# Attention, routed experts and an ELU layer on one core: the finish step of a head moves from slot 4 to slot 5

## The chip, the cores and the metric

The kernel runs on one core of a Trainium2 chip. The metric is the device time of one execution in microseconds (us). The core has a matrix engine (TensorE, PE in the profile, its weight loads shown apart as PEld), a vector engine (VectorE, DVE), a scalar engine (ScalarE, ACT), GpSimd (POOL), and queues that start DMA transfers (SyncE, SP, and others). Each engine works through its own instruction list in order; they meet only at semaphores.

## The reference

Three layers follow one another. The changed lines lie in the first.

```python
q_bits = (np.einsum('bhsd,dk->bhsk', q, proj) > 0)       # 6 hash bits, likewise for k
mask = q_bucket[:, :, :, None] == k_bucket[:, :, None, :]
scores = np.where(mask, scale * np.matmul(q, k.transpose(0, 1, 3, 2)), -1e9)
attn = np.exp(scores - np.max(scores, axis=-1, keepdims=True))
attn = attn / (np.sum(attn, axis=-1, keepdims=True) + 1e-09)
x = np.matmul(attn, v)        # 2 x 8 heads, 768 rows, head width 64; then x is (1536, 512)
# routed layer: argmax over x @ w_gate picks one of 8 experts; relu(x @ w1[e]) @ w2[e], scaled
# last layer: h = x @ w_in; elu(h) @ w_out, 512 -> 2048 -> 512
```

## The kernel before

Attention runs over 16 heads, each of 6 tiles of 128 query rows against all 768 keys: 96 tiles, one per **slot**. Every engine walks the same list of slots: `body(i)` covers a pair of heads, twelve slots `s`, with `j = s // 6` the head of the pair, `u = s % 6` the slot within the head, and `h = i*2 + j`. Pair 0 and pair 7 are written out, pairs 1 to 6 run as a hardware loop, in which some addresses come from registers, and a last short call, `body(PAIRS)`, drains the pipeline. Values are kept as pairs of numbers, a high and a low part, so most products take two or three matmuls.

The work on one tile is spread over the slots. For the tile of slot `s` TensorE writes four score matmuls into `ps_s` (two buffers, lines 564, 565). VectorE finds the row maximum (956), GpSimd makes scale and bias of it in two small steps (432, 434), ScalarE writes `probs` with an exponential and collects the row sums (799). Two slots later TensorE transposes `probs` in two halves of three into `ps_t` (579); ScalarE copies each half to `pt_hi` (790), VectorE forms the low part `pt_lo` (969). `ps_t` has one buffer for each half, so the transposes of a slot wait for `lo_moved` of the slot before (576). The product with V (595, 596) follows for groups of three tiles, in the slots `u` = 5 and 0 and `u` = 2 and 3. ScalarE moves it to `o_sb` at the end of its slots `u` = 0 and `u` = 3 (807).

Beside that, each head prepares the next one through a single bank, `ps_p`: in `u` = 0 and `u` = 1 the next q and k are transposed (`turn_qk`, 529), moved by ScalarE (774) and VectorE (926); in `u` = 2 and 3 they are multiplied by the hash projection (`project`, 535 to 537) and turned to bits (930). The same bank serves the **finish step** of the head before: `finish_head(h - 1)` (twelve matmuls on line 544, two passes of each of six) multiplies `o_sb` by an identity with the gate weights beside it, and VectorE's `move_rows` (940, 942) scales the result by the inverse row sums `inv` into `logit_parts` and `x_rows`. The order of use of the bank is kept by `prep_moved`: each user waits until VectorE has moved what the user before it wrote. So `turn_qk` of `u` = 0 waits for `move_rows` (583). The inverse itself is taken by `reciprocal` (963), after GpSimd has added a small constant to the sums in `u` = 2 (444).

The order inside one slot matters. TensorE: scores, then `turn_qk` of u = 1 or `project`, then the six transposes, then `turn_qk` of u = 0, then the product with V, last the finish step. VectorE: maximum, moves of `ps_p`, `reciprocal`, the two low parts, last `move_rows`. ScalarE: move of q/k for u = 1, the two high parts, move for u = 0, the exponential, the copy to `o_sb`. `FINISH_AT` (244) names the slot of the finish step; `slots_of` (268) uses it for the length of the last short call. The finish step is done in the heads `h` = 1 to 15 for the head before, and once more at the end; heads 1 to 14 also prepare a next head.

After attention VectorE computes the routing, GpSimd scatters the rows, and the expert layer and the last layer follow, each dependent on the one before.

Of the kernel before, what the change touches and what calls it, by code (L numbers as in the profile page):

```python
# [20 lines left out]
def attention_moe_mlp(nc, q, k, v, proj, w_gate, w1, w2, w_in, w_out, out):  # L21
# [59 lines left out]
    with ExitStack() as ctx:  # L81
# [159 lines left out]

        RT_SHIFTED, RT_CHOSEN = 3, 7
        TURN_AT = [2, 5, 8, 11]
        FINISH_AT = 4
        CHUNKS = 4 + 4 * (HEADS - 1) + HEADS

        def chunks_before(h):

            if not isinstance(h, int):
                return h * 5 + 3  # L250
            return 4 if h == 0 else h * 5 + 3 - (4 if h == HEADS else 0)

        def live(i, s, lag, count, per=1):

            if not isinstance(i, int):
                return True
            n = i * SPP + s - lag
            return n >= 0 and n // per < count
# [8 lines left out]
        def slots_of(i):  # L267
            return range(FINISH_AT + 1 if isinstance(i, int) and i == PAIRS else SPP)

        def has_next(i, j):  # L270

            return not isinstance(i, int) or i * 2 + j + 1 < HEADS

        def has_last(i, j):

            return not isinstance(i, int) or i * 2 + j >= 1
# [246 lines left out]
        def _(pe):  # L523
# [24 lines left out]
            def body(i):  # L548
                for s in slots_of(i):
# [35 lines left out]
                    if live(i, s, 5, 2 * HEADS, 3) and (s - 5) % 3 < 2:  # L585
# [11 lines left out]
                        if part == 1:  # L597
                            last.then_inc(weighted, 1)
                    if u == FINISH_AT and has_last(i, j):
                        pe.wait_ge(prep_moved, chunks_before(h) + (4 if has_next(i, j) else 0))  # L600
# [319 lines left out]
        def _(dve):  # L920
            v_ = nc.vector

            def move_qk(j, h, half, bank):
                dve.wait_ge(qk_hi_moved, h * 2 + half + 1)
                cols = slice(half * HW, half * HW + HW)
                v_.tensor_tensor(qk_lo[j][:, cols], bank[:, 0:HW], qk_hi[j][:, cols].bitcast(F32), ALU.subtract).then_inc(prep_moved, 1)

            def move_bits(j, h, half, bank):
                dve.wait_ge(bits_made, h * 2 + half + 1)
                v_.tensor_scalar(bits[:, half * HW:(half + 1) * HW], bank[:, 0:HW], thr[:], amp[:], ALU.is_gt, ALU.mult).then_inc(prep_moved, 1)  # L930

            def move_rows(i, hf):
                dve.wait_ge(inverted, hf + 1)
                dve.wait_ge(finished, hf + 1)
                if not (isinstance(i, int) and i == 0):

                    dve.wait_ge(slots_clear, ST * 16 if isinstance(i, int) and i == PAIRS else i // KD * (16 * (ST - ZEROS_FIRST)) + 16 * ZEROS_FIRST)
                made_rows = ps_p[:, 0:QT * XR].rearrange("p (t c) -> p t c", c=XR)
                scale = inv[:].rearrange("p (t o) -> p t o", o=1)
                v_.tensor_tensor(logit_parts[:, ds(hf % H, 1), ds(hf // H * QT, QT), :].rearrange("p o t e -> p (o t) e"), made_rows[:, :, D:XR],  # L940
                                 scale.to_broadcast([P, QT, E]), ALU.mult).then_inc(logits_moved, 1)
                v_.tensor_tensor(x_rows[:, ds(hf // H * QT, QT), ds(hf % H * D, D)], made_rows[:, :, 0:D],
                                 scale.to_broadcast([P, QT, D]), ALU.mult).then_inc(prep_moved, 1)

            def body(i):
                if isinstance(i, int) and i == PAIRS:
                    dve.wait_ge(logits_moved, H)
                    add_logits(0)
                for s in slots_of(i):
                    n = i * SPP + s  # L950
                    j, u = s // QT, s % QT
                    h = i * 2 + j
                    if live(i, s, 0, UNITS):
                        c = slice(s % 4, s % 4 + 1)
                        dve.wait_ge(scored, n + 1)
                        v_.tensor_reduce(stats[:, 0, c], ps_s[:, 2 * (s % 2):2 * (s % 2) + 2, 0:HW], AX.XY, ALU.max).then_inc(max_found, 1)  # L956
                    if u == 1 and has_next(i, j):
                        move_qk(1 - j, h + 1, u, ps_p)
                    if u in (2, 3) and has_next(i, j):
                        move_bits(1 - j, h + 1, u - 2, ps_p)  # L960
                    if u == 3 and has_last(i, j):
                        dve.wait_ge(guarded, h)
                        v_.reciprocal(inv[:], sums[:, 1 - j]).then_inc(inverted, 1)
                    if live(i, s, 2, UNITS):
                        gb, uu = (s - 2) // 3 % 2, (s - 2) % 3
                        for half in range(2):
                            dve.wait_ge(hi_moved, n * 2 - 4 + half + 1)
                            where = (slice(None), slice(half * HALF, (half + 1) * HALF), slice(uu * P, (uu + 1) * P))
                            v_.tensor_tensor(pt_lo[gb][where], ps_t[:, half, 0:HW].rearrange("p (t c) -> p t c", c=P),  # L969
                                             pt_hi[gb][where].bitcast(F32), ALU.subtract).then_inc(lo_moved, 1)  # L970
                    if u == 0 and has_next(i, j):
                        move_qk(1 - j, h + 1, u, ps_p)
                    if u == FINISH_AT and has_last(i, j):
                        move_rows(i, h - 1)
# [28 lines left out]
            def add_logits(b):  # L1003
                half = slice(b * QT, b * QT + QT)
                return v_.tensor_reduce(LG[:, half], logit_parts[:, :, half].rearrange("p h t e -> p t e h"), AX.X, ALU.add)

            pairs(dve, body)


# [170 lines left out]
```

## Time and profile before

| | |
|---|---|
| three runs | 852.07, 853.45, 855.12 us (median 853.45) |
| the profiled execution | 855.12 us, span from first to last instruction 853.4 us |
| PE busy | 786.0 us (92%), granted clock 0.968 on average |
| PEld, DVE, ACT, POOL busy | 78%, 47%, 40%, 45% of the span |
| first finish step to last finish step | 42.08 to 280.67 us |
| routing product (line 619) | 285.87 us |

Start times are us from the start of the span. A row of a timeline gives start, duration, engine and line, and after "[" how long the engine stood still before it and what released it. Instructions of an engine overlap: the next may start before the one ahead has ended, so the pace is read from start to start.

### The profile page before, as it was taken

The numbers are of one execution on the slowest core, as the hardware profiler recorded it, in microseconds if no ns is written. First come the engines' busy times: TensorE is split into PE (matmuls) and PEld (weight loads), VectorE is DVE, ScalarE is ACT, GpSimd is POOL, SyncE is SP. The second block draws the span as 40 slices with busy tenths as digits, with TensorE's granted clock in tenths as the row PEclk, the third lists the DMA queues.
The fourth block names the chain that finished last, engine by engine and source line by source line (L and its number), as shares of the span: only waits on it lengthen the run. The fifth ranks groups of instructions, "written<-read, shape, count | busy, mean of one in ns | idle before, by whom it ended". The sixth has DMA issues, their size and how long they took to land.

```text
span 853.4 us, 13834 instructions
## 1 busy us (share of the span) xinstructions
PE 786.0 (92%) x4070; PEld 665.1 (78%) x4071; DVE 401.7 (47%) x696; ACT 342.2 (40%) x675; POOL 380.9 (45%) x462
## 2 busy tenths in 40 slices
PE   5899999999999129999999999959999999999998
PEld 4798999999998127888887778737888888888886
DVE  5788888888888402212221212213443433434333
ACT  5778778777777002222222222222322322222221
POOL 3334434434434287799999999059200000000000
PEclk9999999999999659999999999969999999999999
DMA  6466564554451155365565656223000100010001
GB/s 162 105 192 179 130 197 108 129 144 108 113 142 52 61 210 186 123 197 197 186 211 193 205 188 197 75 86 124 25 13 13 49 0 0 0 43 8 1 1 49
DMA packets 70732, 93.87 MB, mean 110 GB/s; under 512 B 32048, under 2 KB 34096, under 8 KB 70704
## 3 DMA queue, kind: packets, MB, share of 16 engines
q1 hardware_dynamic: 62528, 77.06, 30.8%
q10 hardware_dynamic: 6256, 10.16, 3.5%
q0 software_dynamic: 1920, 6.29, 2.2%
q8 instruction: 15, 0.25, 0.1%
q14 instruction: 13, 0.11, 0.0%
HBM read 59.54 MB, written 16.25 MB: 89 GB/s over the span
## 4 chain that ended last, share of the span: by engine, by line
PE 64%; issue 14%; POOL 7%; DMA 6%; DVE 5%; ACT 2%; SPq 1%; DVEq 1%; POOLq 1%; ACTq 0%
PE ps_s L630 9%; PE ps_s L632 9%; PE ps_s L631 9%; PE ps_t L728 5%; PE ps_t L730 5%; PE ps_t L729 5%; PE ps_t L579 5%; POOL w_lo L484 3%; PE ps_p L544 2%; PE ps_s L564 2%; PE ps_s L565 2%; PE ps_o L595 2%; PE ps_o L596 2%; DMA late_stage<-in_moe_w_dram 2%; DVE stats L956 2%
## 5 line engine op out<-in xcount | busy, mean ns | idle before, releaser
L799 ACT ACTIVATE probs<-ps_s,stats 128x768 f32<-128x768 f32 x96 | 95.5, 994 | 41.1 <-POOL stats L434 41.0
L969 DVE TENSOR_TENSOR pt_lo<-ps_t,pt_hi 128x384 fp32r<-128x384 f32 x192 | 97.2, 548 | 8.2 <-ACT pt_hi L790 8.0
L956 DVE TENSOR_REDUCE stats<-ps_s 128x1 f32<-128x768 f32 x96 | 91.6, 954 | 16.7 <-PE ps_s L565 15.4
L790 ACT ACTIVATE pt_hi<-ps_t 128x384 fp32r<-128x384 f32 x192 | 83.8, 490 | 14.3 <-PE ps_t L579 13.6
L484 POOL TENSOR_TENSOR w_lo<-stage,w_hi 128x1024 fp32r<-128x1024 f32 x36 | 86.2, 2393 | 0.0
L484 POOL TENSOR_TENSOR w_lo<-late_stage,w_hi 128x1024 fp32r<-128x1024 f32 x36 | 85.9, 2398 | 0.0
L432 POOL TENSOR_SCALAR stats<-stats 128x1 f32<-128x1 f32 x96 | 21.1, 220 | 140.2 <-DVE stats L956 140.0
L579 PE MATMUL ps_t<-ident,probs 128*128 128x128 f32 x576 | 80.6, 276 | 1.3 <-DVE pt_lo L969 1.2
L728 PE MATMUL ps_t<-yT_hi,w_hi 128*128 (+1 forms) x192 | 77.3, 403 | 2.2 <-DVE yT_lo L1116 1.4
L730 PE MATMUL ps_t<-yT_hi,w_lo 128*128 (+1 forms) x192 | 76.8, 400 | 0.0
L729 PE MATMUL ps_t<-yT_lo,w_hi 128*128 (+1 forms) x192 | 76.6, 399 | 0.0
L630 PE MATMUL ps_s<-w_hi,gT_hi 128*128 128x512 f32 x192 | 76.6, 399 | 0.0
L631 PE MATMUL ps_s<-w_hi,gT_lo 128*128 128x512 f32 x192 | 76.0, 396 | 0.0
L632 PE MATMUL ps_s<-w_lo,gT_hi 128*128 128x512 f32 x192 | 75.9, 395 | 0.0
L896 ACT ACTIVATE elu_e<-elu_e 128x512 f32<-128x512 f32 x48 | 30.3, 632 | 112.2 <-DVE elu_e L1133 112.2
L579 PEld LDWEIGHTS ps_t<-ident,probs 128*128 128x128 f32 x576 | 68.1, 141 | 6.9 <-DVE pt_lo L969 3.5
L564 PE MATMUL ps_s<-key_hi_hi,query_lo_hi 128*128 128x384 f32 x192 | 69.0, 359 | 4.8 <-DMA query_lo_hi<-query_hi_mask 2.4
L1084 DVE TENSOR_TENSOR hidT_lo<-ps_t,hidT_hi 128x512 fp32r<-128x512 f32 x38 | 26.1, 687 | 100.5 <-ACT hidT_hi L840 100.5
L595 PE MATMUL ps_o<-pt_hi,v_split 128*128 128x384 f32 x192 | 70.8, 369 | 1.2 <-DVE pt_lo L969 1.2
L630 PE MATMUL ps_s<-w_hi,xgT_hi 128*128 x152 | 62.9, 414 | 2.9 <-DVE xgT_lo L1078 1.7
L565 PE MATMUL ps_s<-key_lo_mask,query_hi_mask 128*128 128x384 f32 x192 | 65.6, 342 | 0.0
L596 PE MATMUL ps_o<-pt_lo,v_split 128*128 128x384 f32 x192 | 65.2, 339 | 0.0
(151 smaller groups left out, 1612.4 us busy)
## 6 DMA issues: line engine op xcount, KB each, us to landing
stage<-in_moe_w_dram SPq DMA_DIRECT2D x72, 256.0 KB, 2.9
late_stage<-in_moe_w_dram SPq DMA_DIRECT2D x56, 256.0 KB, 2.9
key_hi_hi<-query_hi_mask SPq DMA_DIRECT2D x30, 192.0 KB, 3.8
x_slots<-x_rows SPq DMA_DIRECT2D x19, 256.0 KB, 3.9
xg<-x_slots ACTq DMA_DIRECT2D x19, 256.0 KB, 3.3
y_slots<-y_sb ACTq DMA_DIRECT2D x19, 256.0 KB, 2.9
raw_qk<-in_q_dram SPq DMA_DIRECT2D x16, 192.0 KB, 3.2
raw_v<-in_v_dram SPq DMA_DIRECT2D x16, 192.0 KB, 2.6
```

The costliest lines, as they stand in the source:

```text
L484: g.tensor_tensor(wl[:, ds(at + c * CH, CH)], stages[c % 4].rearrange("p m f -> p (m f)"), wh[:, ds(at + c * CH, CH)].bitcast(F32), ALU.su ...
L579: last = nc.tensor.transpose(ps_t[:, half, t * P:(t + 1) * P], probs[:, (s - 2) % 4, kt * P:(kt + 1) * P], ident[:])
L595: mm(ps_o[:, 0:HW], v2[jv][:, kt].rearrange("p a d -> p (a d)"), pt_hi[gb][:, kt], start=kt == 0, stop=False)
L630: mm(to, x_hi, wh[:, w], start=start, stop=False)
L631: mm(to, x_lo, wh[:, w], start=False, stop=False)
L632: return mm(to, x_hi, wl[:, w], start=False, stop=stop)
L728: mm(ps_t[:, f % 2], wa, ya, start=k == 0, stop=False)
L729: mm(ps_t[:, f % 2], wa, yb, start=False, stop=False)
L730: last = mm(ps_t[:, f % 2], wb, ya, start=False, stop=k == KD - 1)
L799: a(probs[:, s % 4].rearrange("p (h c) -> p h c", h=2), ps_s[:, 2 * (s % 2):2 * (s % 2) + 2, 0:HW], ACT.Exp, bias=stats[:, 2, c], scale=st ...
L956: v_.tensor_reduce(stats[:, 0, c], ps_s[:, 2 * (s % 2):2 * (s % 2) + 2, 0:HW], AX.XY, ALU.max).then_inc(max_found, 1)
L969: v_.tensor_tensor(pt_lo[gb][where], ps_t[:, half, 0:HW].rearrange("p (t c) -> p t c", c=P), pt_hi[gb][where].bitcast(F32), ALU.subtract). ...
```

## The change

The finish step of a head is issued in slot 5 in place of slot 4, on TensorE and on VectorE, and `reciprocal` in slot 4 in place of slot 3. The last short call gets six slots in place of five; the added one holds only the finish step.

```diff
-        FINISH_AT = 4
+        FINISH_AT = 5
...
-                    if u == 3 and has_last(i, j):
+                    if u == 4 and has_last(i, j):
                         dve.wait_ge(guarded, h)
                         v_.reciprocal(inv[:], sums[:, 1 - j]).then_inc(inverted, 1)
```

Unchanged lines that read the constant: 268 (`slots_of`), 599 (TensorE, `finish_head`), 973 (VectorE, `move_rows`).

## Rows read from the trace of the kernel before

**Rows 1.** Waits from 38 to 285 us: waiter, releaser, total us, times, longest.
```profile
PEld ps_p L529 <- DVE query_lo_hi L926: 7.1, 12, 0.7
PEld ps_p L544 <- issue: 4.9, 14, 1.0
```

**Rows 2.** Timeline of TensorE, one head and the step before it.
```profile
116.81 0.42 PE L535 MATMUL ps_p<-query_hi_mask,proj_w 128*128 128x384 f32 x1
...
122.10 0.34 PE L564 MATMUL ps_s<-key_hi_hi,query_lo_hi 128*128 128x384 f32 x1
...
122.80 0.82 PE L579 MATMUL ps_t<-ident,probs 128*128 128x128 f32 x6
123.67 1.55 PE L544 MATMUL ps_p<-finish,o_sb 128*128 x12
125.02 0.42 PE L564 MATMUL ps_s<-key_hi_hi,query_lo_hi 128*128 128x384 f32 x1
...
127.52 0.33 PE L564 MATMUL ps_s<-key_hi_hi,query_lo_hi 128*128 128x384 f32 x1
...
128.87 0.49 PE L529 MATMUL ps_p<-ident,raw_qk 128*128 128x128 f32 x3
129.12 0.42 PE L595 MATMUL ps_o<-pt_hi,v_split 128*128 128x384 f32 x1
...
130.26 0.34 PE L564 MATMUL ps_s<-key_hi_hi,query_lo_hi 128*128 128x384 f32 x1
...
131.51 0.55 PE L529 MATMUL ps_p<-ident,raw_qk 128*128 128x128 f32 x3 [0.39 <-DVE query_lo_hi L926]
...
132.47 0.42 PE L564 MATMUL ps_s<-key_hi_hi,query_lo_hi 128*128 128x384 f32 x1
...
133.27 0.41 PE L535 MATMUL ps_p<-query_hi_mask,proj_w 128*128 128x384 f32 x1
```

**Rows 3.** Timeline of ScalarE in the same head.
```profile
122.02 0.99 ACT L799 ACTIVATE probs<-ps_s,stats 128x768 f32<-128x768 f32 x1 [0.23 <-POOL stats L434]
...
123.00 0.48 ACT L807 ACTIVATE o_sb<-ps_o 128x384 f32<-128x384 f32 x1
...
128.48 0.99 ACT L799 ACTIVATE probs<-ps_s,stats 128x768 f32<-128x768 f32 x1 [1.27 <-POOL stats L434]
...
130.57 1.01 ACT L799 ACTIVATE probs<-ps_s,stats 128x768 f32<-128x768 f32 x1
...
131.54 0.52 ACT L807 ACTIVATE o_sb<-ps_o 128x384 f32<-128x384 f32 x1
...
132.10 0.49 ACT L774 ACTIVATE query_hi_mask<-ps_p 128x384 fp32r<-128x384 f32 x1
```

**Rows 4.** Timeline of VectorE in the same head.
```profile
121.52 0.18 DVE L963 RECIPROCAL inv<-sums 128x6 f32<-128x6 f32 x1
...
123.00 0.96 DVE L956 TENSOR_REDUCE stats<-ps_s 128x1 f32<-128x768 f32 x1 [0.40 <-PE ps_s L565]
123.89 1.02 DVE L969 TENSOR_TENSOR pt_lo<-ps_t,pt_hi 128x384 fp32r<-128x384 f32 x2
...
126.54 0.95 DVE L956 TENSOR_REDUCE stats<-ps_s 128x1 f32<-128x768 f32 x1
...
129.97 1.02 DVE L969 TENSOR_TENSOR pt_lo<-ps_t,pt_hi 128x384 fp32r<-128x384 f32 x2 [0.60 <-ACT pt_hi L790]
130.91 0.55 DVE L926 TENSOR_TENSOR query_lo_hi<-ps_p,query_hi_mask 128x384 fp32r<-128x384 f32 x1
...
132.62 0.56 DVE L926 TENSOR_TENSOR query_lo_hi<-ps_p,query_hi_mask 128x384 fp32r<-128x384 f32 x1 [0.30 <-ACT query_hi_mask L774]
```

**Rows 5.** Timeline of TensorE near the end of attention.
```profile
277.61 0.44 PE L595 MATMUL ps_o<-pt_hi,v_split 128*128 128x384 f32 x1 [1.17 <-DVE pt_lo L969]
```

**Rows 6.** Windows: stretch, length, busy us (count) by engine, granted clock, DMA share, GB/s.
```profile
15.00:38.00 23.00, 19.38 (x111) 16.71 (x110) 17.37 (x28) 16.33 (x35) 10.81 (x26) 0.93 0.44 107
...
240.00:285.00 45.00, 39.31 (x262) 36.19 (x261) 34.48 (x65) 30.69 (x67) 15.87 (x48) 1.00 0.26 73
```

## The prediction

> **What bounds the kernel now.** The page's table of 40 slices comes first: PE is at nine tenths or more through nearly all of attention, so its issue order sets the pace. The waits say what is left over: TensorE stands still before `turn_qk` of slot 1, for VectorE's move of the first half (7.1 us in 12 waits), and before the finish step (4.9 us in 14) [rows 1]. The timeline of one head says how large these are for each head. I write R for the start of its slot 4 scores (122.10), F for the start of the finish step, P for the start of the first projection (slot 2). Before, F = R + 1.57, P = F + 9.60 = R + 11.17, and P to the next R is 116.81 to 122.10, 5.29, without a wait [rows 2]. A head takes 16.46 us. In it are two waits. The transposes of slot 4 need 0.57 but the finish step starts 0.87 after their start, 0.30 late: ScalarE's copy to `o_sb` ends at 123.48, and what is left up to 123.67 is release and register work of the loop [rows 2, 3]. And slot 1: four score matmuls at 0.175 each from 130.26 end the issue at 130.96, `turn_qk` starts at 131.51, 0.55 late [rows 2]. Together 0.85 us per head. The question is whether the moved step removes these or makes others.
>
> **The pieces of TensorE's own work**, read from start to start [rows 2]: scores 0.70 (122.10 to 122.80), and 0.80 where transposes are right ahead of them (132.47 to 133.27); product with V 1.14 (129.12 to 130.26); finish step 1.35 (123.67 to 125.02). Slot 5 is 2.50 (125.02 to 127.52), so its transposes take 2.50 - 0.80 - 1.14 = 0.56. Slot 0 up to `turn_qk` is 1.35, of which the transposes 0.65; `turn_qk` there 0.25; in slot 1 `turn_qk` and transposes 0.96 (131.51 to 132.47). The amount of work does not change: twelve matmuls, one reciprocal and two vector instructions per head are issued one slot later, and no DMA is added or moved. SP's queue waits for chunks of `prep_moved` that come before the moved step; only the times shift. So the price is all in the waits.
>
> **Part 1, slot 4 loses its cover.** Slot 4 has neither a projection nor a product with V, only the finish step, and that now goes. Scores and transposes of slot 4 end at R + 1.26; scores of slot 5 follow at once, since the exponential that they need, slot 3's, started at 122.02 and with its accumulator read is done about R + 1.0 [rows 3]. They end at R + 2.06, and the transposes of slot 5 want `ps_t`. It is free when VectorE has formed the low part of slot 4. That engine takes the maximum of slot 4 at 123.00, R + 0.90, as early as TensorE allows it (its idle 0.40 is put down to the scores), and the low parts 0.89 later [rows 4]. The reciprocal, moved between the two, pushes them: it lasts 0.18, but consecutive vector instructions overlap by 0.07 (0.96 long, 0.89 apart), so I take 0.10 [rows 4]. Low parts start at R + 1.89; they last 1.02 as two, the first done some 0.55 after its start, R + 2.44, the second R + 2.91. A release takes 0.05 (move ends 131.46, TensorE starts 131.51) [rows 2, 4]. So first half at R + 2.49, second at R + 2.96; half of 0.56 on top, R + 3.24; product with V, F' = R + 4.38. Without a wait it would be 0.70 + 0.56 + 0.80 + 0.56 + 1.14 = 3.76; the new wait is 0.62. It hits every head from 1 to 15. Before, the finish step (1.35) and the 0.30 ahead of it covered it.
>
> On that overlap the Trainium skill, VectorE: DVE Perf Modes, section "The DRAIN you can't avoid", says that the next operation starts only when the pipe has emptied. By it the reciprocal would cost its full 0.18, 1.1 us more over 14 heads; the rows here show starts 0.07 before the end ahead, and I go by them.
>
> **Part 2, the finish step's wait goes.** `o_sb` was copied a slot earlier, so of the 0.30 nothing is owed to ScalarE. What the register work leaves is between 0 and the whole 0.30; I take 0, because the wait is met long before and the engine still has matmuls in hand, and keep 0.30 for the range.
>
> **Part 3, the chain behind the finish step now comes nearer to its user.** On VectorE `move_rows` blocks the queue: behind it stood slot 5's maximum, now slot 0's. From F to that maximum 2.87 us pass (123.67 to 126.54) [rows 2, 4]. Two paths go from there.
> - Maximum, low parts 0.89 later, move of q/k half 0 another 0.94 (129.97 to 130.91), `turn_qk` of slot 1 another 0.60 (130.91 to 131.51): F' + 5.30 [rows 2, 4]. TensorE's own work: 1.35 + 0.70 + 0.65 + 0.25 + 1.14 + 0.70 = 4.79. Wait 0.51, against 0.55 before; a part of it may show as `turn_qk` of slot 0 waiting for `move_rows`. From there 0.96 + 0.80 to the projection: F' + 7.06.
> - Maximum, exponential 1.94 later (126.54 to 128.48), copy to `o_sb` 0.97 (130.57 to 131.54), move of q/k half 1 0.56 (to 132.10), projection 1.17 (132.10 to 133.27, through VectorE's move at 132.62): F' + 2.87 + 4.64 = F' + 7.51 [rows 2 to 4]. Before, the exponential in this place was slot 0's too, but its maximum had gone a whole slot after `move_rows`, not right behind it; the blocked one was slot 5's.
>
> The second ends last, 0.45 after the first. P' = R + 4.38 + 7.51 = R + 11.89, against R + 11.17: 0.72 later. In waits: 0.62 + 0.51 + 0.45 = 1.58 against 0.85. From P to the next R TensorE has its 5.29 of work. VectorE and ScalarE enter that stretch late; I let them catch up in it, so that the next maximum of slot 4 is again set by TensorE. If they did not, part 1 would cost more in each head, which keeps the upper side open and is no term.
>
> **Sum.** Heads 1 to 14 have a next head: 14 x 0.72 = 10.1 us. Head 15 prepares nothing; the last tile's maximum no longer stands behind `move_rows`, but TensorE has the finish step 1.35 before the last transposes. Near that end it stands 1.17 for a low part [rows 5]. So between -1.2 and +1.35, and I take 0. Routing, scatter, experts and the last layer depend one on the other and start later by the same amount. The profiled execution would go from 855.12 to 865.2; it is the highest of the three, 1.67 above their median, so the median goes from 853.45 to 863.5. Bounds per head: 0.27 if the second path of part 3 costs nothing (+3.8, 857.2), 1.02 if all register work stays (+14.3, 867.7).
>
> **Rivals.** What can be told from no change is 0.3%, 2.6 us.
> - *Only the transposes wait.* The exponential of slot 0 may start sooner than my chain, since each link is taken from a head in which it was not urgent. Then +0.27 per head: 857.2. Against it: each link is of one engine's own order. Chance 0.20.
> - *The waits go.* Its place is slot 5's transposes. If the low part of slot 4 is done by R + 2.06 (I have 2.44), F' is R + 3.76, and if then only the first path binds, P' = R + 10.82, 0.35 earlier per head, -4.9 us: 848.5; with no wait left at all 10.31, 0.86 earlier, -12.0: 841.4. For it: slot 5's maximum is no longer behind `move_rows`, and rows 1 show 12 us of waits on offer. Against it: VectorE's start at R + 0.90 hangs on TensorE's scores, and 0.89 + 0.10 + 0.55 follow in order. Chance 0.07.
> - *Gain and loss meet.* One of the two new waits only: without that of slot 5, P' = R + 3.76 + 7.51 = 11.27, +0.10, 854.9. This stands also for a change that does little of what it says. Chance 0.07.
> - *The clock falls.* More short stops might lower TensorE's granted clock. From 15 to 38 us, with 19.38 of 23 us busy, it was 0.93; from 240 to 285, with 39.31 of 45, it was 1.00 (2.4 GHz) [rows 6]. Attention after the change is busier than either, about 15.6 of 17.2. At 0.93 throughout the 244 us of attention it would cost 0.07 x 244 = 17 us more: 881. Chance 0.02. The Trainium skill speaks for this one: TensorE: Matmul & The Clock Gate, section "A second HAM failure mode: psum-queue depth-cycling", tells of a kernel whose clock went up and down because of frequent small gaps between groups of matmuls. The rows with gaps here show 1.00.
>
> **How the numbers follow.** The forecast has 0.64: slower, 863.5, by itself 860 to 867. Slower in all: 0.64 + 0.20 + 0.02 = 0.86; within 0.3% 0.07; faster 0.07. The range takes in the first rival and the upper bound: 857 to 868; it leaves out the last three rivals, 0.16, and little of the rest.
>
> **What would show it.** The finish steps of neighbouring heads would be 17.2 us apart, not 16.4. TensorE's wait at line 579 for `pt_lo` would be near 0.6 us per head, where there was next to none; its wait at 535 for line 926 near 0.45 per head; the wait before 544 gone. VectorE's idle before 940 would stay. The routing product would start near 296 in place of 285.87. If 535 does not wait, the first rival holds; if 579 does not wait in slot 5, part 1 is wrong, and with it the sign.

## The result: slower by 0.8%, and the profile after

The changed kernel took 861.14 us (median of 5, 858.0 to 861.51), the kernel before 853.3 (median of 5, 852.07 to 855.12). Over all runs on record (14 of the changed kernel, mean 860.3 us) the ratio is 1.0082, 95% interval 1.0062 to 1.01. The forecast was 863.5 with 857 to 868. The profiled execution took 860.81 us with a span of 859.1, against 855.12 and 853.4.

First the waits of TensorE from 38 to 290 us (waiter, releaser, total us, times, longest), the changed kernel:

```profile
PEld ps_t L579 <- DVE pt_lo L969: 12.4, 34, 0.7
PEld ps_p L535 <- DVE query_lo_hi L926: 5.3, 12, 0.4
...
PEld ps_p L529 <- DVE query_lo_hi L926: 3.2, 12, 0.3
PEld ps_p L529 <- DVE x_rows L942: 2.5, 11, 0.3
PEld ps_p L544 <- issue: 1.1, 1, 1.1
```

The two waits of [rows 1] have shrunk: 7.1 us ahead of line 529 for `query_lo_hi` to 3.2, 4.9 ahead of 544 to 1.1 in one place. Grown are the waits at 579 and 535, to 12.4 and 5.3 us; new are 2.5 us at 529 for `x_rows`. Before, the first two were:

```profile
PEld ps_t L579 <- DVE pt_lo L969: 1.8, 6, 0.7
PEld ps_p L535 <- DVE query_lo_hi L926: 0.6, 2, 0.4
```

Where they lie shows the timeline of TensorE of one head, again from its slot 4 on, as in [rows 2]:

```profile
121.64 0.34 PE L564 MATMUL ps_s<-key_hi_hi,query_lo_hi 128*128 128x384 f32 x1
...
122.34 0.82 PE L579 MATMUL ps_t<-ident,probs 128*128 128x128 f32 x6
122.91 0.42 PE L564 MATMUL ps_s<-key_hi_hi,query_lo_hi 128*128 128x384 f32 x1
...
124.08 1.01 PE L579 MATMUL ps_t<-ident,probs 128*128 128x128 f32 x6 [0.23 <-DVE pt_lo L969]
124.85 0.42 PE L595 MATMUL ps_o<-pt_hi,v_split 128*128 128x384 f32 x1
...
126.00 1.45 PE L544 MATMUL ps_p<-finish,o_sb 128*128 x12
127.25 0.42 PE L564 MATMUL ps_s<-key_hi_hi,query_lo_hi 128*128 128x384 f32 x1
...
131.16 0.55 PE L529 MATMUL ps_p<-ident,raw_qk 128*128 128x128 f32 x3
...
132.12 0.42 PE L564 MATMUL ps_s<-key_hi_hi,query_lo_hi 128*128 128x384 f32 x1
...
133.19 0.45 PE L535 MATMUL ps_p<-query_hi_mask,proj_w 128*128 128x384 f32 x1
...
138.52 0.34 PE L564 MATMUL ps_s<-key_hi_hi,query_lo_hi 128*128 128x384 f32 x1
```

R is 121.64, F' 126.00, P' 133.19, the next R 138.52. The head takes 16.88 us, 0.42 more than the 16.46 of the same head before; the other head of a pair 16.73 against 16.32, 0.41 more (finish steps at 109.27, 126.00 and 142.87 against 107.35, 123.67 and 140.12).

VectorE in the same head, to be read against [rows 4]:

```profile
122.54 0.96 DVE L956 TENSOR_REDUCE stats<-ps_s 128x1 f32<-128x768 f32 x1 [0.46 <-PE ps_s L565]
123.42 0.18 DVE L963 RECIPROCAL inv<-sums 128x6 f32<-128x6 f32 x1
123.51 0.98 DVE L969 TENSOR_TENSOR pt_lo<-ps_t,pt_hi 128x384 fp32r<-128x384 f32 x2
...
128.06 0.21 DVE L940 TENSOR_TENSOR logit_parts<-ps_p,inv 128x48 f32 x1 [1.05 <-PE ps_p L544]
128.29 0.56 DVE L942 TENSOR_TENSOR x_rows<-ps_p,inv 128x384 f32 x1
128.77 0.95 DVE L956 TENSOR_REDUCE stats<-ps_s 128x1 f32<-128x768 f32 x1
...
130.56 0.55 DVE L926 TENSOR_TENSOR query_lo_hi<-ps_p,query_hi_mask 128x384 fp32r<-128x384 f32 x1
...
132.58 0.56 DVE L926 TENSOR_TENSOR query_lo_hi<-ps_p,query_hi_mask 128x384 fp32r<-128x384 f32 x1 [0.37 <-ACT query_hi_mask L774]
```

And ScalarE, against [rows 3]:

```profile
130.71 0.99 ACT L799 ACTIVATE probs<-ps_s,stats 128x768 f32<-128x768 f32 x1 [0.72 <-POOL stats L434]
131.60 0.19 ACT L799 ACTIVATION_READ_ACCUMULATOR probs<-ps_s,stats 128x1 f32 x1
131.69 0.48 ACT L807 ACTIVATE o_sb<-ps_o 128x384 f32<-128x384 f32 x1
132.06 0.49 ACT L774 ACTIVATE query_hi_mask<-ps_p 128x384 fp32r<-128x384 f32 x1
```

The chain through this head is the one that the prediction drew, some links of it waits and some an engine's own order: maximum of slot 4, reciprocal, low part, transposes, product, finish step, `move_rows`, maximum of slot 0 (128.77), exponential (130.71), copy (131.69), move (132.06), low part of q/k (132.58), projection (133.19).

**Where the span's 5.7 us are.** From R of head 1 to R of head 15: 226.87 us before (40.73 to 267.60), 232.72 after (38.08 to 270.80), +5.85, that is 14 x 0.42. From there to the routing product: 18.27 against 19.89, +1.62. Head 1 began 2.65 earlier, in slots that the change does not touch: TensorE had waited 2.39 us for a DMA before and 1.12 here, and started the scores behind that wait at 28.56 and 27.54, 1.02 earlier. The other 1.63 are TensorE's clock. From these scores to R of head 1 the same instructions took 12.17 us before and 10.54 here, and the granted clock of the kernel before was 0.50 in the stretch 29.2 to 32.6. Window 28 to 34 (length, busy us of PE, PEld, DVE, ACT and POOL, granted clock, DMA), first before, then after:

```profile
28.00:34.00 6.00, 5.44 (x26) 5.31 (x27) 2.69 (x5) 2.93 (x6) 1.95 (x4) 0.72 0.01 3
```

```profile
28.00:34.00 6.00, 6.00 (x44) 5.71 (x44) 5.06 (x9) 4.98 (x12) 3.51 (x7) 1.00 0.16 35
```

After the routing product 567.5 against 568.4, +0.9. Sum: 5.85 + 1.62 - 2.65 + 0.9 = 5.7. The changed heads and the drain without its clock give 5.85 + 0.24 = 6.1; the two falls of the clock, one in each profile, nearly cancel.

Of the 1.62 the larger part is TensorE's clock. Windows of the last product with V, with the same columns, first before, then after:

```profile
278.00:280.00 2.00, 1.99 (x12) 1.67 (x10) 0.00 (x0) 0.00 (x0) 0.00 (x0) 1.00 0.00 0
```

```profile
281.00:283.00 2.00, 1.95 (x7) 1.95 (x8) 0.09 (x1) 0.00 (x0) 0.00 (x0) 0.65 0.00 0
```

The granted clock fell to its lower level, 1.2 GHz, from some 281.5 to 285. The twelve matmuls of that product went from start to start in 2.05 us before (277.61 to 279.66) and 3.25 after (281.05 to 284.30), and the first finish matmul came 0.2 later behind them: 1.4 us.

### The profile page after: what moved, and what is told of

It reads as the page before. It is cut to its first block, busy times and chain, and to the rows that moved or that the text cites. A ratio compares the mean times of both kernels' runs of the same rounds, so it can differ in the third digit from the quotient of the medians.

```text
span 859.1 us, 13834 instructions
## 1 busy us (share of the span) xinstructions
PE 791.8 (92%) x4070; PEld 664.0 (77%) x4071; DVE 400.7 (47%) x696; ACT 342.6 (40%) x675; POOL 380.7 (44%) x462
## 4 chain that ended last, share of the span: by engine, by line
PE 59%; issue 18%; POOL 7%; DVE 6%; DMA 5%; ACT 2%; POOLq 1%; SPq 1%; DVEq 1%; ACTq 0%
PE ps_s L630 8%; PE ps_s L631 8%; PE ps_s L632 8%; PE ps_t L728 5%; PE ps_t L730 5%; PE ps_t L729 5%; PE ps_t L579 4%; PE ps_o L595 3%; PE ps_o L596 3%; POOL w_hi L480 3%; POOL w_lo L484 2%; DVE stats L956 2%; PE ps_p L544 2%; DMA late_stage<-in_moe_w_dram 2%; PE ps_s L564 2%
## 5 line engine op out<-in xcount | busy, mean ns | idle before, releaser
L579 PE MATMUL ps_t<-ident,probs 128*128 128x128 f32 x576 | 82.6, 277 | 5.1 <-DVE pt_lo L969 5.0
L579 PEld LDWEIGHTS ps_t<-ident,probs 128*128 128x128 f32 x576 | 66.2, 141 | 16.9 <-DVE pt_lo L969 14.1
```

The source lines that it names most:

```text
L579: last = nc.tensor.transpose(ps_t[:, half, t * P:(t + 1) * P], probs[:, (s - 2) % 4, kt * P:(kt + 1) * P], ident[:])
```

## The experiments

The theory: (a) the finish step had covered the wait of slot 5's transposes for slot 4's low part; (b) behind the finish step the chain through VectorE and ScalarE now ends at the next projection. The rivals were that only one of the two matters, that an added instruction costs wherever it stands, and that ScalarE's order does not matter. Each run was taken beside the kernel before (its medians 853.7 to 853.8). A pair of heads, from finish step to finish step, took 32.76 us before and 33.60 after; this can be read to 0.02 and tells more than the total.

**e1: the reciprocal alone.** From the kernel before:

```diff
-                    if u == 3 and has_last(i, j):
+                    if u == 4 and has_last(i, j):
```

> The kernel before with the reciprocal alone moved to slot 4, the finish step left in slot 4. Theory (lost cover in slot 5 and the chain behind move_rows): the low part of slot 4 comes 0.09 us later, but nothing waits for it there, since VectorE then waits for the finish step anyway. Finish steps stay 16.31 and 16.45 us apart; 852 to 856 us. Rival (each instruction added ahead of the low part costs, cover or not): 0.09 us per head, pairs of heads 32.94 in place of 32.76 us, +1.3 us.

Measured: 853.18 us in one run, a pair of heads 32.78. The 0.02 is no more than can be read: the reciprocal costs nothing where VectorE waits for the finish step behind it.

**e5: the reciprocal back, the finish step in slot 5.** From the changed kernel:

```diff
-                    if u == 4 and has_last(i, j):
+                    if u == 3 and has_last(i, j):
```

> The changed kernel with the reciprocal put back into slot 3, the finish step left in slot 5. Theory: the low part of slot 4 starts 0.09 us earlier, the transposes of slot 5 that wait for it and the finish step behind them too, and so does the projection at the end of the chain: pairs of heads 33.61 - 2 x 0.09 = 33.43 us, 1.3 us in all; 859.5. Rival (the reciprocal is hidden): 33.61 as it is.

Measured: 859.19 us in one run, a pair 33.52. So 0.04 per head, half of what was expected. VectorE:

```profile
123.28 0.96 DVE L956 TENSOR_REDUCE stats<-ps_s 128x1 f32<-128x768 f32 x1 [0.40 <-PE ps_s L565]
124.17 1.02 DVE L969 TENSOR_TENSOR pt_lo<-ps_t,pt_hi 128x384 fp32r<-128x384 f32 x2
```

The pair of low parts starts right behind the maximum, 0.89 after it, but takes 1.02; behind the reciprocal it started 0.97 after it and took 0.98. Half of the reciprocal hides in that. Of the loss of 0.42 per head the reciprocal's move carries a tenth.

**e2: the finish step ahead of the transposes of slot 5.** From the changed kernel, on TensorE:

```diff
+                    if u == FINISH_AT and has_last(i, j):
+                        pe.wait_ge(prep_moved, chunks_before(h) + (4 if has_next(i, j) else 0))
+                        finish_head(h - 1)
                     if live(i, s, 2, UNITS):
                         for half in range(2):
...
-                    if u == FINISH_AT and has_last(i, j):
-                        pe.wait_ge(prep_moved, chunks_before(h) + (4 if has_next(i, j) else 0))
-                        finish_head(h - 1)
```

> The changed kernel with the twelve finish matmuls of slot 5 put ahead of the slot's transposes in place of last. Theory: they cover the 0.38 + 0.19 us for which the transposes of slot 5 wait for the low part of slot 4, and they end 1 us earlier, so that move_rows does not hold up the maximum of slot 0. From R: finish step at R + 2.06, transposes R + 3.4, product R + 4.0, VectorE's maximum of slot 0 at R + 6.1, projection near R + 10.5; heads 15.9 us apart on average in place of 16.8; 14 x -0.9 = -13 against the changed kernel, 847 us, faster than before. Rival (move_rows directly ahead of slot 0's maximum is what costs, the place on TensorE does not matter): the wait at 579 in slot 5 may go, but heads stay about 16.8 apart, 861 us.

Measured: 845.82 us, ratio to before 0.9919 (0.9893 to 0.9944): faster than both. TensorE (the transposes have line 582 here) and VectorE, R at 118.02:

```profile
120.07 1.46 PE L544 MATMUL ps_p<-finish,o_sb 128*128 x12
121.36 0.82 PE L582 MATMUL ps_t<-ident,probs 128*128 128x128 f32 x6
121.94 0.42 PE L598 MATMUL ps_o<-pt_hi,v_split 128*128 128x384 f32 x1
...
128.51 0.44 PE L535 MATMUL ps_p<-query_hi_mask,proj_w 128*128 128x384 f32 x1
```

```profile
122.42 1.02 DVE L969 TENSOR_TENSOR pt_lo<-ps_t,pt_hi 128x384 fp32r<-128x384 f32 x2 [0.68 <-ACT pt_hi L790]
123.38 0.21 DVE L940 TENSOR_TENSOR logit_parts<-ps_p,inv 128x48 f32 x1
...
124.09 0.95 DVE L956 TENSOR_REDUCE stats<-ps_s 128x1 f32<-128x768 f32 x1
```

The finish step starts at R + 2.05, the transposes at R + 3.34 without a wait, `move_rows` without a wait behind the low parts, the maximum of slot 0 at R + 6.07, the projection at R + 10.49 (expected 2.06, 3.4, 6.1, 10.5). Pairs of heads are 31.5 us apart. `move_rows` stands directly ahead of slot 0's maximum here too; so that alone is not the loss. e2 gives back the cover and starts the finish step earlier in one edit, so it shows the two together and not the share of each.

**e3: TensorE as before, `move_rows` behind the maximum of slot 5.** From the changed kernel, the first change on TensorE, the second on VectorE, where the lines go from the end of the slot:

```diff
-                    if u == FINISH_AT and has_last(i, j):
+                    if u == FINISH_AT - 1 and has_last(i, j):
...
                         v_.tensor_reduce(stats[:, 0, c], ...).then_inc(max_found, 1)
+                    if u == FINISH_AT and has_last(i, j):
+                        move_rows(i, h - 1)
```

> TensorE as before (finish step at the end of slot 4), but VectorE does move_rows in slot 5 behind its maximum; the reciprocal in slot 4. Theory: the cover is kept, so no wait at 579; VectorE no longer stands 0.8 to 0.9 us idle ahead of move_rows, its maximum of slot 5 comes 0.5 us earlier, and the 0.55 us wait of turn_qk in slot 1 goes; the 0.30 ahead of the finish step stays. 14 x -0.5 = -7 us against before: 846. Rival (VectorE's queue is not what holds turn_qk; the copy and exponential on ScalarE are): the wait stays, within 2 us of before. Second rival (the whole loss lies in the chain behind move_rows, none in the cover): the same -7, so it is e2 that tells these two apart.

Measured: 849.96 us, ratio 0.9955 (0.9937 to 0.9972), about half of the expected gain; a pair of heads 32.13 where no DMA was waited for, 32.48 at most, in place of 32.76. The wait ahead of 529 fell from 7.1 to 0.9 us as expected, but one at 535 took its place (waits, 38 to 290 us):

```profile
PEld ps_p L544 <- issue: 4.9, 14, 1.0
...
PEld ps_p L535 <- DVE query_lo_hi L926: 3.8, 12, 0.4
...
PEld ps_p L529 <- DVE query_lo_hi L926: 0.9, 6, 0.2
```

I had counted the wait that goes and not the next one on the same chain. The 4.9 us at 544 stay, as the finish step is in slot 4.

**e4: on ScalarE the copy to `o_sb` behind the move of q/k.** From the changed kernel (`copy_o` holds the unchanged lines of the copy, 801 to 807):

```diff
                     if u == 1 and has_next(i, j):
                         move_qk(1 - j, h + 1, u, ps_p)
+                    if u == 1:
+                        copy_o(s - 1)
...
-                    if live(i, s, 6, 2 * HEADS, 3) and (s - 6) % 3 == 0:
...
+                    if u == 3:
+                        copy_o(s)
```

> The changed kernel with one swap on ScalarE: in slot 1 the move of q/k half 1 comes ahead of the copy to o_sb of slot 0. Theory (the chain maximum, exponential, copy, move, projection ends last, 0.27 us behind the other): the projection's wait of 0.46 us (133.19 against 132.12 + 0.80) shrinks by 0.27, then the other chain binds; 14 x -0.27 = -3.8 us against the changed kernel, 857.3. Rival (the projection waits for VectorE's own queue, not for ScalarE): no change, 861.

Measured: 861.56 us, ratio 1.0087 (1.0069 to 1.0105); a pair 33.58, nothing gained. But the waits changed (38 to 290 us):

```profile
PEld ps_t L579 <- DVE pt_lo L976: 18.2, 60, 0.7
...
PEld ps_p L535 <- DVE query_lo_hi L933: 0.2, 1, 0.2
```

The 5.3 us at 535 are gone, and 579 has 5.8 more: the transposes of slot 2 now wait for the low part of slot 1, whose high part stands behind the copy on ScalarE. Neither theory had said this; the copy had only been moved one link along the chain.

**e10: the copy behind the high parts of slot 1.** As e4, with `copy_o(s - 1)` placed behind the loop over the two high parts.

> The changed kernel with ScalarE's copy to o_sb of slot 0 put behind the high parts of slot 1. In e4 it went between the move of q/k and the high parts, the projection's wait went and the transposes of slot 2 waited as much for the low part: the copy's 0.37 us stayed in the chain, one step on. Theory: behind the high parts it is out of the chain, so projection and transposes both come 0.27 us earlier, where TensorE's other chain binds: 14 x -0.27 = -3.8 us, 857.3. Rival (the chain does not end at ScalarE but at VectorE's total work in slots 1 and 2): no change, 861.

Measured: 856.07 us, ratio to before 1.003 (1.0016 to 1.0043), 5.1 below the changed kernel by the medians and 4.3 by the means of all runs; a pair 32.96, 0.32 less per head against an expected 0.27. ScalarE and TensorE:

```profile
130.02 0.49 ACT L774 ACTIVATE query_hi_mask<-ps_p 128x384 fp32r<-128x384 f32 x1
130.41 0.87 ACT L800 ACTIVATE pt_hi<-ps_t 128x384 fp32r<-128x384 f32 x2
131.15 0.51 ACT L786 ACTIVATE o_sb<-ps_o 128x384 f32<-128x384 f32 x1
```

```profile
131.18 0.42 PE L535 MATMUL ps_p<-query_hi_mask,proj_w 128*128 128x384 f32 x1
...
131.79 0.85 PE L579 MATMUL ps_t<-ident,probs 128*128 128x128 f32 x6
```

Projection and transposes follow without a wait. So part (b) of the theory is worth 0.32 of the 0.42 per head, as the difference of these two kernels. The waits at 579 stay in e10 (12.1 us). No run gives back the cover alone; that the other 0.10 are its net price is a subtraction, not a measurement.

**e7 and e11: is there more on top of e2?** e7 puts `move_rows` behind the maximum of slot 5 in e2, e11 takes the copy of e10 into e2.

> As e2 (finish step ahead of the transposes of slot 5), and VectorE does move_rows right behind the maximum of slot 5, in the 0.68 us for which it waits there for the high part. Theory: the maximum of slot 0 comes 0.4 us earlier, so the wait of the projection of slot 2, 0.26 us per head in e2, goes; 14 x -0.26 = -3.6 us against e2: 842. Rival (the projection's wait is set on ScalarE by other work than the exponential of slot 0): as e2, 846.

> e2 with the copy of e10. Theory: the projection's 0.26 us wait in each head goes, TensorE then works without a wait through a head: 15.5 us apart in place of 15.76, -3.6 us against e2, 842. Rival as for e10: as e2, 846.

Measured: e7 846.39 us (0.9916, 0.9894 to 0.9938), e11 845.43 (0.9905, 0.9887 to 0.9924), e2 845.82: no difference that these runs can tell. In e7 the wait at 535 went from 5.0 only to 4.3 us, where its theory had it gone, and the time did not fall: the theory failed. In e11 it fell from 5.0 to 0.3, and many heads are 15.49 us apart, but in others another wait appears, for the DMAs that place the next head's operands (waits, 38 to 282 us):

```profile
PE ps_s L564 <- DMA query_lo_hi<-query_hi_mask: 1.5, 3, 0.8
PEld ps_s L564 <- issue: 1.4, 3, 0.6
```

The DMAs may be the next bound; this was not followed further.

## Why the prediction was right, step by step

**Part 1 (new wait in slot 5), right.** Transposes at R + 2.44 (said 2.49), product at R + 3.21 (3.24), F' = R + 4.36 (4.38). The reciprocal's term was 0.10; undone alone it is worth 0.04 (e5). The low parts start 0.09 after the reciprocal's start, which lasts 0.18, so they do not wait for it to end. The prediction took from the Trainium skill (VectorE: DVE Perf Modes, "The DRAIN you can't avoid") only the sentence that the next operation waits for an empty pipe. The same paragraph adds that a next operation which is not held starts earlier, and the starts here agree with that.

**Part 2 (the wait ahead of the finish step goes), right.** The product starts at 124.85 and the finish step at 126.00, 1.15 later: no wait, no register work in sight.

**Part 3 (the chain at the projection), right in kind, too large in size.** The first path to `turn_qk` took 5.16 (said 5.30). The second, which ends last as said, took 7.19, not 7.51. Two links are off. From the finish step to the maximum of slot 0 it is 2.77, not 2.87: the twelve matmuls take 1.25 of TensorE, not the 1.35 of [rows 2], where the finish step had stood in a wait. In head 1 of the kernel before it stands behind transposes too, but starts without a wait, and there they took 1.26:

```profile
41.42 0.82 PE L579 MATMUL ps_t<-ident,probs 128*128 128x128 f32 x6
42.08 1.46 PE L544 MATMUL ps_p<-finish,o_sb 128*128 128x72 f32 x12
43.34 0.42 PE L564 MATMUL ps_s<-key_hi_hi,query_lo_hi 128*128 128x384 f32 x1
```

And from the copy to the move of q/k it is 0.37, not 0.56: in the row that I took it from, 131.54 to 132.10, the move had waited for `turn_qk` of slot 1 (131.51, 0.55 long, ends 132.06). A start-to-start time holds a wait of its own, if there is one. The rest of the difference is 0.03. P' is R + 11.55, not 11.89, and with 5.33 in place of 5.29 up to the next R the head is 0.42 longer, not 0.72. In waits of TensorE per head: 0.60 for the low part, 0.47 up to `turn_qk` of slot 1 and 0.27 more up to the projection, 1.34 (said 1.58), against 0.85 before, with 0.10 taken off by the shorter finish step and 0.04 added behind the projection.

**The stretch from P to the next R, left as an open point, right.** It took 5.33. But it had little to spare in slot 2: in e4, where the copy stands ahead of the high part of slot 1, its transposes wait.

**Sum.** 14 x 0.42 = 5.9 in place of 10.1. Head 15 and the drain, taken as 0 within -1.2 and +1.35, cost 0.2 without the clock's 1.4. The medians differ by 7.8, the ratio says 7.0 (5.3 to 8.5 us), the two profiled executions differ by 5.7, since that of before was 1.8 over its median, with the DMA wait and the clock's fall near its start in it. 5.9 + 0.2 is inside the interval. The rest seems to go with the clock: of the 14 runs of the changed kernel those with a mean granted clock of 0.972 took 858.1 us (3 runs), those with 0.966 took 861.6 (5 runs); the kernel before, in the 28 runs beside the experiments, took 852.9 at 0.972 (13 runs) and never went as low as 0.966. At 0.972 the two are 5.3 apart, over all of these runs 6.5. Where the clock fell in the runs without a profile is not known. So part of the forecast's closeness is luck: 2.4 us off the median, it had 4.2 us too much in the heads and no term for the drain's clock.

**Rivals.** The first (only the transposes wait, +0.27 per head) is nearly what e10 makes: +0.10 per head without the second path. *The waits go* failed at its own point: the low part was not there by R + 2.06. It had its merit, though. e2 meets that condition by other means, and takes 8 us off. *Gain and loss meet* did not come: both new waits are there. The clock rival was wrong in its place: 1.00 through the heads, a fall only in the drain. Its price was read from an average, too: the 0.93 of [rows 6] is no steady level, but 1.00 with a fall to 0.50 from 29.2 to 32.6, behind the DMA wait.

**The signs.** Finish steps are 16.8 us apart on average, not 17.2; the waits at 579 and 535 are where they were said to be, the latter 0.44 each; the wait before 544 is gone but for one; VectorE's idle before 940 stays (1.05, before 0.91); the routing product starts at 290.69, not 296, as head 1 had begun 2.65 earlier and each head grew by 0.42.

## What to carry to other kernels

When a block of work moves in an in-order engine, ask what it stood in front of: here 1.35 us of finish step had covered what became a 0.6 us loss at the transposes of slot 5, and putting the same block ahead of transposes and product in its new slot (e2) turned a loss of 7.8 us into a gain of 8. Draw the chain behind the moved step up to the next engine that has no slack, and when one link is taken out, look for the link behind it (e3, e4) before counting the gain. A link's time is taken from a row in which the instruction did not wait.

## What the runs showed that was not expected

TensorE's granted clock fell to 1.2 GHz in the drain of attention in 2 of the 4 profiles with the finish step last in slot 5 (the changed kernel and e4; not e5 and e10), and in none of the 6 others at that place. Near the start, at 29 us, it fell in 2 of the 10 profiles (the kernel before and e11), behind waits for a DMA of 2.39 and 2.08 us, and stayed at 1.00 in others behind waits of 2.26, 2.35 and 2.57 us. Ahead of the fall in the drain the engine had been partly busy only: in the changed kernel 0.88 of 2 us from 279 to 281, with waits of 0.34 and 1.17 us. Before, with 0.83 of 2 us and a wait of 1.17 likewise, it did not fall. What tips it these runs don't tell; where it fell, the drain took 10.13 and 10.14 us from finish step to finish step, where not, 8.73 and 8.76.

VectorE stands 1.05 us ahead of `move_rows`, though the twelve matmuls end at 127.45 (126.00 + 1.45) and it starts at 128.06, 0.61 later. Over the twelve heads of the loop this is 0.48 to 0.63 us, in the four finish steps of the written-out pairs and the last call 0.09 to 0.11. The trace has two register instructions on line 940 for each head of the loop (24 in all, 0.05 to 0.27 us each) and none elsewhere, so the address work of the loop, done once the wait is met, is the likely cause; no run takes it out. In e2 VectorE reaches `move_rows` behind its low parts, 1.8 us after the matmuls have ended, and does not stand idle there.
